# Gated linear attention with two feed-forward stages: a shorter level, another start order, one mixing tile a slot, and a last output by tiles

## The reference

```
f = sigmoid(f_logit)                      # gates, per token and channel
state = f[t] * state + outer(k[t], v[t])  # per head, for t in 768 tokens
y[t] = q[t] @ state
x = y by token, [4, 768, 384]
h = x.T @ U @ V ; u = x + h.T             # mixing over tokens, rank 32
x = u + relu(u @ w_ch1) @ w_ch2           # 384 -> 1536 -> 384
h = relu(x @ w_in)                        # 384 -> 1024
c = conv over 3 tokens of h, per channel
out = (h * sigmoid(c)) @ w_out            # 1024 -> 384
```

## Time and profile before

| | |
|---|---|
| median of 3 runs | 715.05 us |
| lowest and highest | 713.25 and 716.5 us |
| the profiled execution, its own time | 715.21 us |
| its span, first to last instruction | 713.4 us |
| TensorE busy | 684.9 us (96%) |
| VectorE busy | 438.8 us (62%) |
| GpSimd busy | 266.1 us (37%) |
| ScalarE busy | 248.8 us (35%) |

### The profile page before, as it was taken

The page is one execution under the profiler, slowest core; times in us unless marked ns, Lnnn a source line. Parts: engine busy times, 40 slices in busy tenths (PEclk is TensorE's granted clock), DMA queues, the critical chain, the costliest instruction groups (busy, mean ns, idle before and its releaser), DMA issues.

```text
span 713.4 us, 22514 instructions
## 1 busy us (share of the span) xinstructions
PE 684.9 (96%) x10076; PEld 648.7 (91%) x10076; DVE 438.8 (62%) x744; ACT 248.8 (35%) x508; POOL 266.1 (37%) x243
## 2 busy tenths in 40 slices
PE   2888999999999999999999999999999999999997
PEld 1788799999999999999999899999999989999997
DVE  6886675674786764364597855365498651122875
ACT  1034534251355412223245432213145541121553
POOL 4872574463542333152263315143263220030432
PEclk9999999999999999999999999999999999999999
DMA  9331444432002111201201110200000100000000
GB/s 207 94 93 37 113 135 118 118 90 62 8 18 74 35 34 25 68 4 28 64 2 56 46 57 3 68 24 25 24 2 2 35 34 1 0 1 1 1 34 33
DMA packets 22719, 33.46 MB, mean 47 GB/s; under 512 B 3584, under 2 KB 15616, under 8 KB 22624
## 3 DMA queue, kind: packets, MB, share of 16 engines
q1 hardware_dynamic: 21616, 30.27, 15.4%
q10 hardware_dynamic: 1008, 1.77, 1.1%
HBM read 27.31 MB, written 4.72 MB: 45 GB/s over the span
## 4 chain that ended last, share of the span: by engine, by line
PE 91%; POOL 2%; DVE 2%; issue 2%; ACT 1%; DMA 1%; ACTq 0%; POOLq 0%; DVEq 0%
PE acc L751 8%; PE att L614 7%; PE hb L732 7%; PE acc L752 7%; PE acc L756 7%; PE hb L733 7%; PE hb L734 7%; PE acc L790 5%; PE hb L771 5%; PE hb L773 5%; PE hb L772 5%; PE acc L791 5%; PE acc L795 5%; PE att L660 3%; PE att L636 1%
## 5 line engine op out<-in xcount | busy, mean ns | idle before, releaser
L1138 DVE SCALAR_TENSOR_TENSOR r_lo<-hb,r_hi 128x386 fp32r<-128x386 f32 (+1 forms) x96 | 53.5, 557 | 179.1 <-ACT r_hi L914 179.1
L914 ACT ACTIVATE r_hi<-hb 128x386 fp32r<-128x386 f32 (+1 forms) x96 | 47.2, 491 | 248.8 <-PE hb L734 248.8
L1227 POOL TENSOR_TENSOR k_t<-k_t,blocks 112x512 f32<-112x512 f32 x60 | 81.2, 1356 | 135.0 <-PE att L614 127.2
L1266 POOL TENSOR_TENSOR r_lo<-conv,r_hi 128x384 fp32r<-128x384 f32 x64 | 63.3, 989 | 141.6 <-ACT r_hi L929 141.6
L751 PE MATMUL acc<-r_hi,w_ch_hi 128*128 128x386 f32 (+1 forms) x288 | 103.1, 358 | 0.0
L732 PE MATMUL hb<-u_hi,w_ch_hi 128*128 128x386 f32 (+1 forms) x288 | 98.1, 341 | 1.2 <-POOL w_ch_lo L1239 0.7
L733 PE MATMUL hb<-u_hi,w_ch_lo 128*128 128x386 f32 (+1 forms) x288 | 97.5, 339 | 0.0
L752 PE MATMUL acc<-r_hi,w_ch_lo 128*128 128x386 f32 (+1 forms) x288 | 97.3, 338 | 0.0
L734 PE MATMUL hb<-u_lo,w_ch_hi 128*128 128x386 f32 (+1 forms) x288 | 96.9, 336 | 0.0
L1168 DVE SCALAR_TENSOR_TENSOR conv<-hb,convw,conv 128x384 f32<-128x384 f32 x128 | 79.1, 618 | 4.5
L614 PEld LDWEIGHTS att<-q_t,k_t 48*64 48x64 f32 (+3 forms) x3840 | 59.3, 134 | 19.0 <-issue 13.2
(11 more groups left out here) (147 smaller groups left out, 1258.0 us busy)
## 6 DMA issues: line engine op xcount, KB each, us to landing
v_p<-in_vn_dram SPq DMA_DIRECT2D x12, 384.0 KB, 3.7
out_dram<-ostage SPq DMA_DIRECT2D x24, 192.0 KB, 2.1
q_t<-in_qT_dram SPq DMA_DIRECT2D x21, 192.0 KB, 3.5
k_t<-in_kT_dram SPq DMA_DIRECT2D x21, 192.0 KB, 3.4
gates<-in_fT_dram SPq DMA_DIRECT2D x21, 192.0 KB, 3.6
ostage<-in_w_ch_dram SPq DMA_DIRECT2D x14, 192.0 KB, 2.6
conv<-in_w_ch_dram SPq DMA_DIRECT2D x10, 192.0 KB, 3.0
ostage<-in_w_out_dram SPq DMA_DIRECT2D x5, 192.0 KB, 2.4
```

## The change

- Levels 1 and 2 (blocks of 2 and 4) leave out the key columns of the last block, which no later query of the group meets: 62 and 60 columns in place of 64. Levels 3 to 5 did so before.
- In the last slot, output tiles 0 and 1 get their high products, then their low ones; tile 2 gets all three of its products after them. Its store is issued from ScalarE's queue, right behind the copy, and has a semaphore of its own.
- In the loads of the first three duos the gates come first, then q, then k, on both queues; the masks and the identity are issued behind the loads of duo 0. GpSimd clears gates ahead of k, and clears two of the three scores tiles. VectorE makes the masks after the first step EVEN.
- For duos 0 and 1 the even keys are scaled on VectorE, ahead of the even queries; GpSimd waits only for the gates and merges them.
- Mixing tiles 3, 4, 5 come in slots 0, 1, 2; before, 3 in slot 0, 4 and 5 in slot 1.

```diff
@@ -116,8 +116,8 @@
         for s in range(2 * N1 + 2 * N2):
             if s < 2 * N1:
                 order.append(("first1", b, s))
-                if s < 2:
-                    order += [("mix", b, CT + i) for i in ([0], [1, 2])[s]]
+                if s < CT:
+                    order.append(("mix", b, CT + s))
             else:
                 order += [("states", n) for n, st in at.get(s - 1, []) if st == U]
                 order.append(("first2", b, s - 2 * N1))
@@ -165,6 +165,10 @@
     return {t: i + 1 for i, t in enumerate(t for t in ORDER if kinds(t))}
 
 
+
+EARLY_K = 2
+
+
 def by_vector(n, st):
 
     return st < LEVELS - 2 or (st == LEVELS - 2 and n >= DUOS)
@@ -176,7 +180,7 @@
 TAKEN_AT = numbered(lambda t: t[0] == "att" and t[2] >= 0 and by_vector(t[1], t[2]))
 QUARTER_AT = numbered(lambda t: t[0] == "att" and t[2] == LEVELS - 2 and not by_vector(t[1], t[2]))
 LAST_AT = numbered(lambda t: t[0] == "att" and t[2] == LEVELS - 1)
-GATED_AT = numbered(lambda t: t[0] == "att" and t[2] < LEVELS and t[2] != 0)
+GATED_AT = numbered(lambda t: t[0] == "att" and t[2] < LEVELS and t[2] != 0 and not (t[1] < EARLY_K and t[2] == EVEN))
 PAIRED_AT = numbered(lambda t: t[0] == "att" and t[2] in (EVEN, 1))
 MERGED_AT = numbered(lambda t: t[0] == "att" and 2 <= t[2] < LEVELS)
 T_AT = numbered(lambda t: t[0] == "att" and t[2] == T)
@@ -390,7 +394,8 @@
         loaded_v = [sem(f"loaded_v{i}") for i in range(3)]
         loaded_masks, loaded_mix, loaded_conv = sem("loaded_masks"), sem("loaded_mix"), sem("loaded_conv")
         loaded_w = [sem(f"loaded_w{i}") for i in range(STAGES)]
-        stored, tile_done, last_copied = sem("stored"), sem("tile_done"), sem("last_copied")
+        stored, stored_last = sem("stored"), sem("stored_last")
+        tile_done, last_copied = sem("tile_done"), sem("last_copied")
         cleared_q, cleared_k, cleared_s = sem("cleared_q"), sem("cleared_k"), sem("cleared_s")
         masks_ready, padded = sem("masks_ready"), sem("padded")
         vstack_hi, vstack_ready = sem("vstack_hi"), sem("vstack_ready")
@@ -400,6 +405,7 @@
         level_done, level_taken = sem("level_done"), sem("level_taken")
         quarters_taken, last_taken = sem("quarters_taken"), sem("last_taken")
         q_ready, k_ready, pairs_ready = sem("q_ready"), sem("k_ready"), sem("pairs_ready")
+        k_first_ready = sem("k_first_ready")
         merged_ready = sem("merged_ready")
         turned, k_end_ready = sem("turned"), sem("k_end_ready")
         update_done, decay_done, state_ready = sem("update_done"), sem("decay_done"), sem("state_ready")
@@ -437,6 +443,13 @@
             elif st > 2:
                 engine.wait_ge(merged_ready, merged(n, st - 1))
 
+        def k_gated(engine, n, st):
+
+            if st == 0 and n < EARLY_K:
+                engine.wait_ge(k_first_ready, n + 1)
+            else:
+                engine.wait_ge(k_ready, gated(n, st))
+
         def weights_split(engine, n):
 
             engine.wait_ge(w_lo_done, low_halves(n, False))
@@ -454,7 +467,7 @@
         def _(sp):
             def load_k(n):
                 if set_before(n) is None:
-                    sp.wait_ge(cleared_k, 2 * n + 1)
+                    sp.wait_ge(cleared_k, 2 * n + 2)
                 else:
                     sp.wait_ge(turned, turns(set_before(n)))
                 b, j = n // DUOS, n % DUOS
@@ -464,7 +477,7 @@
 
             def load_f(n):
                 if set_before(n) is None:
-                    sp.wait_ge(cleared_k, 2 * n + 2)
+                    sp.wait_ge(cleared_k, 2 * n + 1)
                 else:
                     sp.wait_ge(q_ready, scaled(set_before(n), 0))
                     sp.wait_ge(pairs_ready, paired(set_before(n), 0))
@@ -475,7 +488,7 @@
 
             def load_q(n):
                 if q_before(n) is None:
-                    sp.wait_ge(cleared_q, q_of(n) + 1)
+                    sp.wait_ge(cleared_q, q_of(n) + 1 + (q_of(n) == DUOS))
                 else:
                     sp.wait_ge(y_done, outputs(q_before(n)))
                 b, j = n // DUOS, n % DUOS
@@ -513,16 +526,17 @@
                     sp.dma_start(convw[:, j * h:(j + 1) * h, :],
                                  conv_w[:, j * h:(j + 1) * h, :]).then_inc(loaded_conv, 16)
 
-            consts()
             for task in ORDER:
                 kind = task[0]
                 if kind == "load":
                     n = task[1]
                     if n == DUOS - 1:
                         sp.wait_ge(q_ready, scaled(0, EVEN))
+                    load_f(n)
                     load_q(n)
                     load_k(n)
-                    load_f(n)
+                    if n == 0:
+                        consts()
                 elif kind == "piece":
                     if task[1] + AHEAD < len(PIECES):
                         piece(task[1] + AHEAD)
@@ -564,13 +578,16 @@
                 elif kind == "out":
                     _, b, part = task
                     for t in range(3):
+                        if (b, part, t) == (B - 1, 1, 2):
+                            continue
                         if last_out(b, part, t):
                             sp.wait_ge(last_copied, 1)
                         else:
-                            sp.wait_ge(out_copied, 6 * b + 3 * part + t + 1 - (b == B - 1 and part == 1 and t == 2))
+                            sp.wait_ge(out_copied, 6 * b + 3 * part + t + 1)
                         q = 3 * part + t
                         sp.dma_start(out[b, q * P:(q + 1) * P, :], ostage[:, t, :]).then_inc(stored, 16)
-            sp.wait_ge(stored, 16 * 6 * B)
+            sp.wait_ge(stored, 16 * (6 * B - 1))
+            sp.wait_ge(stored_last, 16)
 
         @block.tensor
         def _(pe):
@@ -597,14 +614,14 @@
                                   sums[rows][:, :, ch, :], start=True, stop=True, skip_group_check=True)
                 if st < LEVELS:
                     c = 1 << st
-                    pe.wait_ge(k_ready, gated(n, max(st - 1, 0)))
+                    k_gated(pe, n, max(st - 1, 0))
                     if st > 0:
                         pe.wait_ge(q_ready, scaled(n, st - 1))
                         if by_vector(n, st - 1):
                             pe.wait_ge(level_taken, taken(n, st - 1))
                         else:
                             pe.wait_ge(quarters_taken, quarters(n))
-                    left, half = C - c if st >= 3 else C, 32 if st == 0 else 0
+                    left, half = C - c if st >= 1 else C, 32 if st == 0 else 0
                     for u in range(2):
                         for r in range(PAIRS):
                             for par, ch in QUADRANTS:
@@ -780,7 +797,8 @@
                 if b == 0 and part == 0:
                     weights_split(pe, PIECE_AT["out", j, 0])
                 wh, wl = wsplit["out"]
-                for t in range(3):
+                last = (b, q) == (B - 1, 2 * N2 - 1)
+                for t in range(2 if last else 3):
                     o, ts = acc[:, t, 0:DM], slice(t * P, (t + 1) * P)
                     if j == 0:
                         if part == 1:
@@ -792,6 +810,9 @@
                 pe.wait_ge(g_lo_ready, 2 * N2 * b + q + 1)
                 for t in range(3):
                     o, ts = acc[:, t, 0:DM], slice(t * P, (t + 1) * P)
+                    if last and t == 2:
+                        pe.matmul(o, r_hi[:, s, ts], wh[:, j, :], start=False, stop=False)
+                        pe.matmul(o, r_hi[:, s, ts], wl[:, j, :], start=False, stop=False)
                     mm = pe.matmul(o, r_lo[:, s, ts], wh[:, j, :], start=False, stop=(j == N2 - 1))
                     if j == N2 - 1 and t < 2:
                         mm.then_inc(tile_done, 1)
@@ -821,15 +842,15 @@
                 odd = slice(C, C + D)
                 if n == DUOS - 1:
                     act.wait_ge(q_ready, scaled(0, EVEN))
+                act.wait_ge(cleared_k, 2 * n + 1)
+                act.dma_start(gates[n][odd, :].rearrange("d (u t) -> d u t", u=2),
+                              fT[0, 2 * n:2 * n + 2, 1].rearrange("u d t -> d u t")).then_inc(loaded_f[n], 16)
                 act.wait_ge(cleared_q, n + 1)
                 act.dma_start(q_t[n][odd, :].rearrange("d (u t) -> d u t", u=2),
                               qT[0, 2 * n:2 * n + 2, 1].rearrange("u d t -> d u t")).then_inc(loaded_q[n], 16)
-                act.wait_ge(cleared_k, 2 * n + 1)
+                act.wait_ge(cleared_k, 2 * n + 2)
                 act.dma_start(k_t[n][odd, :].rearrange("d (u t) -> d u t", u=2),
                               kT[0, 2 * n:2 * n + 2, 1].rearrange("u d t -> d u t")).then_inc(loaded_k[n], 16)
-                act.wait_ge(cleared_k, 2 * n + 2)
-                act.dma_start(gates[n][odd, :].rearrange("d (u t) -> d u t", u=2),
-                              fT[0, 2 * n:2 * n + 2, 1].rearrange("u d t -> d u t")).then_inc(loaded_f[n], 16)
 
             def sigmoid_gates(n):
```

(33 more changed lines are left out.)

16 lines of the change are left out of this document (8 added, 8 removed).

## The result

| | before | after |
|---|---|---|
| median, 20 runs each on one chip | 714.37 us | 712.62 us |
| lowest and highest | 712.41, 717.05 | 709.79, 715.76 |
| the profiled execution: own time, span | 715.21, 713.4 | 713.61, 711.8 |

The ratio is 0.9972, 95% interval 0.996 to 0.9984: some 2 us faster, less than the 0.5% that was called the bound. Run again later, on another chip, the changed kernel gave 0.9959 (0.9943 to 0.9974). The forecast was 710.0 us, and faster by over 0.5% was held the likeliest; 712.62 lies near the upper end of its range, within 0.5% of before. Where 5.2 us were to come, 1.6 came between the two profiled executions.

What follows compares the result with a forecast made beforehand. TensorE, busy 96% of the span, was taken as the bound, except in the first 76 us, where it waits for GpSimd and VectorE. 0.9 + 1.3 + 2.7 + 0.3 = 5.2 off 715.21 gave 710.0 us, range 707.5 to 713.0.

Steps and rivals of the forecast that it cites:

- Shorter levels: Levels 1 and 2: six fewer key columns a duo save 0.74 us in nine later duos, 0.16 in duo 2; together 0.9.
- Mixing a tile a slot: Slots 0 to 2 of each batch: TensorE's waits at L732 and in batch 0 go; 1.3 us, bounds 0 and 1.6.
- Rival 2: Mixing gives nothing: the gap at L732 only moves to mix 5 or the next attention step; 711.3 us, chance 0.1.
- the wait goes: 0.4: Batch 0: VectorE's job for mix 5 moves behind duo 3's level 1, so TensorE's 0.37 us wait for scores ends; 0.4.
- The start: First 76 us: gates loaded first and early keys on VectorE bring the chain forward 2.7 us, bounds 1.2 and 3.6.
- k last, at some 14.2 ... the masks behind duo 0's loads cost SP's queue two issues, under duo 1's: Loads at the start: duo 1's k lands at some 14.2 us, wanted at 15.1; the moved masks cost only two issues.
- signs of being wrong: L1051 starting after 9.7 us, duo 2's key scaling less than 2 us earlier, or batch 1 under 2 us earlier.
- rival 1: At the start VectorE, given GpSimd's job, slows beside it; only 1.2 of 2.7 us arrive: 711.5 us, chance 0.15.
- Behind that nothing in the first 76 us waits for a fixed time: After duo 2's keys, loads and weight pieces shift along with level counts, so the whole 2.7 us gain is kept.
- rival 3: More comes: TensorE's gaps after 38 us close too as GpSimd is relieved; up to 1.5 more, 708.5 us, chance 0.12.
- Rival 4: Slower: TensorE's rate rises later or falls again at 76 to 90 us; 718.4 us for 12 us of work, chance 0.04.
- The end: Last slot: tile 2's store issues right after its copy, no longer behind two issues on SP; 0.3 us, bounds -0.2 and 0.6.

Runs made afterwards that it cites:

- c64: The changed kernel with 64 key columns again in level 1 of duo 3 alone; 712.86 us in one timed run.
- mix: The kernel before with only the mixing of tiles 3, 4, 5 one a slot; 714.14 us, ratio 0.9976 to before.
- masks_first: The changed kernel with the masks and identity issued ahead of duo 0's loads again, as before; 711.46 us, ratio 0.9942 to before.
- masks_early1: masks_first with only duo 0's first k scaled on VectorE, duo 1's on GpSimd; 710.66 us, ratio 0.9932 to before; again 711.57 us, 0.9936.
- best: masks_early1 with 64 key columns again in level 1 of duo 3; 711.83 us, ratio 0.9939 to before.

## Why the prediction was wrong

- **Shorter levels**: right. 0.70 us against 0.74 in the nine duos behind 82 us; levels 1 and 2 take 1.11 and 1.08 us. The 0.16 us of duo 2 can't be told from the scatter before 82 us. By the rule of the Trainium skill (TensorE: Matmul & The Clock Gate, section LDWEIGHTS (loading the stationary operand)) 2.9 us were to come; the trace does not agree for these overlapping loads.
- **Mixing a tile a slot**: the mechanism is right and the term was too small, 1.78 instead of 1.3 us. Rival 2 falls. But in batch 0 of the whole change 1.06 of it is lost again (9.78 us from the first stage-one product to the first of its second form, 8.72 in c64). The step that failed is "the wait goes: 0.4": alone it went (mix), in the whole change it grew from 0.37 to 1.02 us. The step asked whether TensorE's wait for scores would lose its cause, not whether VectorE's job ahead of them could meet GpSimd's.
- **The start**: forecast 2.7 us, 0.8 at duo 2's keys and 0.13 at 81.5 us. The first steps were right to 0.3 us (10.93 for 11.2, 15.01 for 15.3, GpSimd's keys of level 1 at 17.04 for 17.3). The step that failed is "k last, at some 14.2 ... the masks behind duo 0's loads cost SP's queue two issues, under duo 1's". It counted the issues and not the transfers: they held the queue 3.8 us, k came at 16.0, and with that VectorE lost its lead over GpSimd. With the masks first the 2.5 us are there at duo 2's keys. Two of the signs of being wrong that were named came true: duo 2's keys less than 2 us earlier (0.8), and batch 1, forecast 2.8 to 3.1 us earlier, starts at 247.56 instead of 247.26 us, 0.3 later. This is rival 1's outcome by another cause: VectorE is slowed beside GpSimd, but only because k is late.
- **"Behind that nothing in the first 76 us waits for a fixed time"**: wrong. TensorE's gaps for instructions do. Its gaps grew from 1.9 to 2.8 us, and in the first execution the mixing's products took 0.6 longer (2.61 for 2.01) as the rate rose inside them. This is no loss of the change but chance: over executions it costs or gives 2 us. With it, rival 3's closing of the gaps after 38 us fell too; they opened. Rival 4, TensorE's rate falling again, is a real thing (five of fourteen profiles), but executions of before have it as well, and it is in neither profile of after: it doesn't come with the change each time.
- **The end**: 0.13 for 0.3; the last product came 0.19 later, the store 0.32 earlier.

Sum between the profiled executions: 0.13 (to 81.5 us) + 1.16 (to the last product: 0.70 + 1.78 - 0.19, less 1.1 at the meeting) + 0.32 = 1.6 us, which is the difference of the spans. How much of the start's gain many runs keep is less sure: masks_first's ratio stands 0.0030 and 0.0017 below the two of after, 2.1 and 1.2 us, about the 1.7 to 1.9 that it gains at duo 2's keys; the intervals are as wide as that.

The fastest version is masks_early1: 0.9932 and 0.9936 of before on two chips, some 4.7 us. Beside the changed kernel on one chip it was 1.8 us below it, but the two intervals overlap (0.9911 to 0.996, 0.9943 to 0.9974), so that this much is likely and not shown.

## What to carry to other kernels

A load of many small packets moved to the middle of a queue, while another queue is at work, is paid in transfer time by everything behind it: read landings, not issues, and put small tables first if nothing but their own few tenths stands behind. Where two engines that slow each other are released by the same event, ask which of them begins first and who stands behind the other; a gain of hundredths elsewhere can turn that round. And before gains at a start are added up, look whether a waiting engine is short of data or of its own program.

## What the runs showed of the hardware

- **VectorE against GpSimd**: the one that is clearly first keeps its speed and the other pays: VectorE 0.68 or 0.69 and GpSimd 1.82 to 1.89 us when GpSimd starts at most 0.018 us ahead, 1.79 to 1.83 and 1.31 when it is 0.021 to 0.062 ahead; alone 0.69 and 1.3. The second ends nearly its own length after the first: VectorE 0.54 us after GpSimd in best, GpSimd 1.19 us after VectorE in c64. The Trainium skill says this (SBUF — State Buffer, section SBUF: two separate sides): whoever starts first holds the shared ports for the whole instruction. The rows agree.
- **Bytes don't price a load**: 160 KB of masks and identity held SP's queue for 3.8 us (8.1 to 11.9), where 192 KB of k had taken 1.5 (q landed at 6.6, k at 8.1). It takes two things together: many small packets (256 of 768 and 512 bytes, against 96 of 2 KB) and another queue at work. From 8.1 to 11.9 us SP's queue passed 305 packets with 0.30 MB and ScalarE's 260 with 0.47 MB; with ScalarE's queue idle the same 256 packets took 1.3 us. That the queues take turns packet by packet is inferred from these counts.
- **TensorE can run out of instructions** (inferred, not tried directly): gaps of up to 2.15 us (mix, at 53 us) at fixed counts of its program, 127 or 128 products apart or a multiple of 127, when it runs through many small products; they moved with dummies at its start, and ended 1.1 to 1.8 us after a packet of 16 KB on the queue for instructions.
- **TensorE's rate** rose between 60 and 76 us in executions of one kernel, with nothing in the program changed, and in five of fourteen profiles it fell again between 70 and 82 us. What decides it stays open.
